# A recurrent attention and two mixing layers on one core: the opening loads, its first and last update of T and K, and its state products rewritten

## The reference

```python
for t in range(S):
    state = alpha[t][:, None] * state + outer(k[t], v[t])   # 48 x 48 per head
    y[t] = q[t] @ state
```

```python
xk = mu_k * x + (1 - mu_k) * x_prev;  xr = mu_r * x + (1 - mu_r) * x_prev
x = sigmoid(xr @ w_r) * (relu(xk @ w_k) ** 2 @ w_v)         # 384 -> 1024 -> 384
u = x + (x^T @ U @ V)^T                                     # over tokens, rank 32
out = u + relu(u @ w_ch1) @ w_ch2                           # 384 -> 1536 -> 384
```

## Time and profile before

| | |
|---|---|
| median of 3 runs | 734.57 us |
| lowest and highest run | 734.43, 735.68 us |
| the profiled execution: its time, its span | 734.48 us, 732.7 us |
| TensorE matmul, share of the span | 96% |
| VectorE, ScalarE, GpSimd | 57%, 35%, 8% |
| DMA, mean over the span | 55 GB/s |

### The profile page before, as it was taken

One profiled execution on the slowest core, in us unless ns is written; L12 is line 12 of the kernel. 1 busy time (PEld: TensorE's weight loads), 2 busy tenths in 40 slices (PEclk: granted clock), 3 DMA queues, 4 the chain that ended last, 5 costly groups with the idle time before them and its releaser, 6 DMA issues.

```text
span 732.7 us, 21764 instructions
## 1 busy us (share of the span) xinstructions
PE 700.2 (96%) x9800; PEld 671.6 (92%) x9800; DVE 416.3 (57%) x731; ACT 259.4 (35%) x516; POOL 62.4 (9%) x123
## 2 busy tenths in 40 slices
PE   4769979999999999999999999999999999999998
PEld 4668968999999999999999999999999998989998
DVE  4788788763874268661885339652685515331312
ACT  1445655324423243243424144243334235321211
POOL 3401101001010011000110010100111000000000
PEclk9969999999999999999999999999999999999999
DMA  8655320023001221024000231023000001000000
GB/s 233 210 196 174 97 86 3 2 90 86 34 4 46 71 59 41 2 58 117 33 4 1 70 105 39 2 59 106 15 32 3 1 10 38 1 1 1 32 1 33
DMA packets 17565, 40.23 MB, mean 55 GB/s; under 512 B 2336, under 2 KB 8480, under 8 KB 17472
## 3 DMA queue, kind: packets, MB, share of 16 engines
q1 hardware_dynamic: 17408, 38.77, 17.5%
q10 hardware_dynamic: 64, 0.07, 0.0%
HBM read 32.93 MB, written 4.72 MB: 51 GB/s over the span
## 4 chain that ended last, share of the span: by engine, by line
PE 90%; DVE 5%; ACT 2%; issue 1%; DMA 1%; SPq 0%; POOL 0%; DVEq 0%; ACTq 0%
PE acc L662 13%; PE hps L662 13%; PE acc L663 13%; PE acc L664 13%; PE hps L664 11%; PE hps L663 11%; PE aps L473 4%; PE aps L636 2%; PE aps L617 2%; PE aps L594 1%; PE aps L484 1%; PE aps L572 1%; DMA QK<-in_q 1%; PE aps L491 1%; DVE QK L1143 1%
## 5 line engine op out<-in xcount | busy, mean ns | idle before, releaser
L1368 DVE SCALAR_TENSOR_TENSOR hid_l<-hps,hid_h 128x384 fp32r<-128x384 f32 x96 | 53.4, 556 | 189.1 <-ACT hid_h L1029 188.6
L1029 ACT ACTIVATE hid_h<-hps 128x384 fp32r<-128x384 f32 x96 | 47.2, 491 | 208.9 <-PE hps L664 208.7
L662 PE MATMUL hps<-in_h,w_h 128*128 128x384 f32 x288 | 98.8, 343 | 0.8 <-DVE in_l L1350 0.8
L664 PE MATMUL hps<-in_h,w_l 128*128 128x384 f32 x288 | 96.9, 336 | 0.0
L663 PE MATMUL hps<-in_l,w_h 128*128 128x384 f32 x288 | 96.8, 336 | 0.0
L663 PE MATMUL acc<-w_l,hid_h 128*128 128x384 f32 x288 | 96.8, 336 | 0.0
L662 PE MATMUL acc<-w_h,hid_h 128*128 128x384 f32 x288 | 96.6, 335 | 0.0
L664 PE MATMUL acc<-w_h,hid_l 128*128 128x384 f32 x288 | 96.4, 335 | 0.0
L1143 DVE TENSOR_TENSOR QK<-QK,T 112x768 f32<-112x768 f32 x80 | 77.0, 971 | 12.4 <-PE aps L473 10.1
L1496 POOL TENSOR_TENSOR T<-T 112x384 f32<-112x384 f32 (+4 forms) x80 | 43.9, 551 | 457.0 <-DVE QK L1143 231.3
L991 ACT ACTIVATE tmp<-hps 128x384 f32<-128x384 f32 x64 | 31.5, 492 | 134.7 <-PE hps L664 134.5
(11 more groups left out here) (134 smaller groups left out, 1228.5 us busy)
## 6 DMA issues: line engine op xcount, KB each, us to landing
QK<-in_k SPq DMA_DIRECT2D x16, 336.0 KB, 4.2
QK<-in_q SPq DMA_DIRECT2D x16, 336.0 KB, 5.2
T<-in_alpha SPq DMA_DIRECT2D x16, 336.0 KB, 4.3
vt<-in_v SPq DMA_DIRECT2D x16, 288.0 KB, 3.2
raw<-in_w_ch SPq DMA_DIRECT2D x6, 768.0 KB, 6.7
out<-x SPq DMA_DIRECT2D x24, 192.0 KB, 1.9
QK<-in_q_odd SPq DMA_DIRECT2D x16, 168.0 KB, 4.1
raw_k<-in_w_k SPq DMA_DIRECT2D x3, 512.0 KB, 4.6
```

The costliest lines, as they stand in the source:

```text
L662: pe.matmul(o, a[0], b[0], start=first, stop=False)
L664: return pe.matmul(o, a[1], b[0], start=False, stop=last)
L1029: nc.scalar.activation(hid[0][:, f % 2, :], hps[f % 2][:, 0:HT], ACT.Relu).then_inc(s_rel2, 1)
L1368: nc.vector.scalar_tensor_tensor(out=hid[1][:, f % 2, :], in0=hps[f % 2][:, 0:HT], scalar=0.0, in1=hid[0][:, f % 2, :].bitcast(F32), op0=A ...
```

## The change

Only the opening (unit 0) is changed, apart from where the low part of V is made.

- The loads of K, Q and T for both g no longer bring the 16 rows between the heads: each of the six is now two of 48 rows, the second head's issued by SyncE and the first head's by ScalarE. VectorE first zeroes rows 32 to 63 of the six tiles, and each of ScalarE's DMAs waits for one of these. The two loads of odd queries become four of 48 rows.
- Level 0 of T is multiplied by VectorE instead of GpSimd.
- The last doubling is four instructions of half the size, K for both g and then Q for both g; `turn_k` waits for K alone, `T_end` for both.
- `end_chunks(0)` goes by the order of the three copies and waits for one at a time; it writes to four banks, one of them of another group, and needs no bank a second time.
- `from_states(0)` waits for 9 of the 11 instructions of `end_states`, that is not for `carry`; the first level of unit 1 waits for all 11.
- One of three copies of the result on VectorE is made by ScalarE, as the last of its own; VectorE's second low part of w_k moves behind its two remaining copies.
- V lands in another place, and its low part is made by VectorE beside the first layer's last step.

```diff
+def first_loads(g):
+    u = units[0]
+    return ((part(u.K(), g), k[0, 0, g], s_ldk[g]), (part(u.Q(), g), q[0, 0, g], s_ldq[g]),
+            (part(u.T[0:HR], g), alpha[0, 0, g], s_lda[g]))
 # SyncE
-            for g in range(2):
-                sp.dma_start(part(K, g), k[0, 0, g]).then_inc(s_ldk[g], 16)
-                sp.dma_start(part(Q, g), q[0, 0, g]).then_inc(s_ldq[g], 16)
-                sp.dma_start(part(T[0:HR], g), alpha[0, 0, g]).then_inc(s_lda[g], 16)
+            for g in range(2):
+                for to, src, done in first_loads(g):
+                    sp.dma_start(to[HS:HR, :], src[HS:HR, :]).then_inc(done, 16)
...
+            sp.wait_ge(s_vst, 3)
             load_part(w2w, w_ch2, 0, F2 // 3, s_w2[2])
 # ScalarE, at its very start
+            for g in range(2):
+                for i, (to, src, done) in enumerate(first_loads(g)):
+                    act.wait_ge(s_zero, 3 * g + i + 1)
+                    act.dma_start(to[0:D, :], src[0:D, :]).then_inc(done, 16)
 # VectorE, at its very start
+            for g in range(2):
+                for to, _, _ in first_loads(g):
+                    nc.vector.memset(to[W2:HS, :], 0.0).then_inc(s_zero, 1)
 # TensorE
             def end_chunks(n):
+                if opens(n):
+                    kept(pe, n, ML, 1)
+                    kept(pe, n, LV, 1)
+                    for j in range(2 * NC):
+                        m, c = j // HC, j % HC
+                        if j % NP == 0:
+                            pe.wait_ge(s_kt, j // NP + 1)
...
             def from_states(n):
-                pe.wait_ge(s_st, st_count(n + 1))
+                pe.wait_ge(s_st, 2 * NT - 3 if opens(n) else st_count(n + 1))
 # VectorE
+            def last_doubles(n):
+                u, l = unit(n), LV - 1
+                for side, of, done in ((left, u.K, s_qk), (right, u.Q, (s_last, s_last))):
+                    for g in range(2):
+                        dve.wait_ge(s_lv[g], (LV - 1) * n + l)
+                        dve.wait_ge(s_T[g], LV * n + l)
...
+                        nc.vector.tensor_tensor(x, x, by, ALU.mult).then_inc(done[g], 1)
...
                         if opens(n):
+                            t_odd, t_even = (x(part(unit(n).T[0:HR], g), 0) for x in (right, left))
+                            dve.wait_ge(s_Ke[g], 1)
+                            nc.vector.tensor_tensor(t_odd, t_odd, t_even, ALU.mult).then_inc(s_T[g], 1)
                             double(n, 0, g)
...
-                nc.vector.tensor_copy(
-                    xT[0:D, 1:KT, 1:1 + HT],
-                    y_all[rows, 2 * HT:].rearrange("p (i t) -> p i t", t=HT)).then_inc(s_xe, 1)
...
                 low(NR)
+                keep_odd(0)
                 low(NR + 1)
-                keep_odd(0)
```

More of the change, by code:

```diff
@@ L197, in ds_block @@
         def ds_block(n, c, z):
+            if opens(n):
+                i, at = (((0, 0), (0, NP * D), (1, 0)), ((2, 0), (2, NP * D), (4, 0)))[z][c]
+                return opening[i][:, at:at + NP * D]
             i, at = (((0, 0), (0, NP * D), (1, 0)), ((1, NP * D), (2, 0), (2, NP * D)))[z][c]
[L199 removed]
+            return aps[i][:, at:at + NP * D]
         def place(y):
@@ L515, in levels @@
                         loaded(pe, n, s_ldk, g)
+                        if g == 0 and n == 1:
+                            pe.wait_ge(s_st, st_count(1))
                         if g == 0 and n == 2:
@@ L606, in own_chunks @@
                 pe.wait_ge(s_kt, kx_count(n + 1))
-                if n > 0:
+                if not opens(n):
                     pe.wait_ge(s_st, st_count(n + 1))
@@ L1143, in double @@
                 nc.vector.tensor_tensor(qk, qk, t, ALU.mult).then_inc(s_qk[g], 1)
+            def last_doubles(n):
[4 more added lines that the diff above has]
+                        dve.wait_ge(s_T[g], LV * n + l)
+                        B, x = 1 << l, side(part(of(), g), l)
+                        t_end = u.T[0:HR, g * S:(g + 1) * S]
+                        at = B - 1 if side is right else 2 * B - 1
+                        by = t_end[:, at:S:2 * B].unsqueeze(2).to_broadcast([HR, S // (2 * B), B])
+                        nc.vector.tensor_tensor(x, x, by, ALU.mult).then_inc(done[g], 1)
             def update_k(n, g):
@@ L1202, in levels @@
                 for l in range(2, LV):
+                    if opens(n) and l == LV - 1:
+                        last_doubles(n)
+                        yield
+                        return
                     for g in range(2):
@@ L1420, in finish_first @@
                 mix(0, 1, 0, lambda: next(first_gate))
-            channel_mix(0, 0, step, FIRST_DVE, finish_first)
+            channel_mix(0, 0, step, FIRST_DVE, finish_first, v_low)
             run(steps)
@@ L1482, in attention @@
                 t = unit(n).T[0:HR]
-                for l in range(LV):
+                for l in range(1 if opens(n) else 0, LV):
                     B = 1 << l
```

57 lines of the change are left out of this document (32 added, 25 removed).

## The result

| | before | after |
|---|---|---|
| median of 9 runs each, same chip | 735.52 us | 737.60 us |
| least, most | 734.43, 737.03 | 735.72, 738.55 |
| profiled execution | 734.48 us (span 732.7) | 735.72 us (span 734.0) |

The ratio is 1.0026, 95% interval 1.0014 to 1.0037: the changed kernel is slower by 0.26%, and the interval lies clear of 1. Forecast were 732.3 us and a range of 730.5 to 733.9.

A forecast was written before the change was run, and what follows sets the result against it. The opening's dependency chain up to the mix was taken as the bound, TensorE being busy and unchanged from 100 us. Terms -0.2 - 0.3 - 0.93 - 0.75 = -2.2 took 734.5 to 732.3 us, range 730.5 to 733.9.

The forecast's parts named there:

- Loads: Opening loads of 96 rows for 112: second Q lands earlier, less zeroing delay; -0.2 us, bounds -1.05 and +0.6.
- rival of slow loads: Opening: twelve 48-row transfers at half rate, second Q landing at 16.9, total 739.6 us; chance 0.05.
- T on VectorE: Opening, level 0: product of T takes 0.57 on VectorE, right behind its update of K; -0.3 us.
- K first and state matmuls by copies: Last doubling to state matmuls: K ready earlier, matmuls no longer wait for third copy; -0.93 us, bounds -0.6 and -1.2.
- Nine instead of eleven: State chain: from_states waits for nine end_states instructions, own_chunks ending at the same moment, 37.5; another -0.75 us.
- third rival: Pause in own_chunks stays at 37.35, ended by something outside the chain; only -0.7, or 733.8 us; chance 0.10.
- Moved copies: Result copies and low parts moved between engines hide in idle time, ScalarE's extra copy under a DMA wait; 0 us.
- The clock: TensorE's granted clock, falling at 38.9 and back at 52.5 in the opening, could change the forecast time.
- first rival: Clock stays at 2.4 GHz through from_states, which saves 1.1; total 731.0 us; chance 0.22.
- second rival: Clock still rises at 52.5, so 2.2 us more of the gate run at half speed; 733.4 us; chance 0.17.
- The test given in the prediction: Mix on VectorE should start at 43.9 instead of 46.06; forecast wrong if it moved by less than 1.5 us.

The follow-up runs named there:

- 48 rows on one queue: Changed kernel with all twelve loads of 48 rows on SyncE, each first head's load behind its zeroing; 735.15 us.
- old loads: Changed kernel with its opening loads as in the kernel before: full 112 rows, all on SyncE, no zeroing; 735.05 us.
- Q before alpha: Changed kernel with old loads, K and Q of both groups issued ahead of both alpha loads; 735.25 us.
- w_v held: Changed kernel with old loads, SyncE's first load of w_v held until own_chunks finished its first group; 734.68 us.
- `end_chunks` as before: Changed kernel with old loads, end_chunks(0) again behind all three copies, in the old order and banks; 735.79 us.
- odd rows behind Q: Changed kernel, SyncE issuing the four odd-query loads only once both halves of the second Q have landed; 737.77 us.
- 32 in front: 32 small matmuls on constants at TensorE's start, spread over four array corners: changed kernel with old loads 733.72 us, kernel before 735.28 us.
- 32 in front, Q first: Changed kernel with old loads and 32 small matmuls at TensorE's start, K and Q of both groups issued ahead of alpha; 733.81 us.

## Why the prediction was wrong

The forecast was 2.2 us faster, and measured were 2.1 us slower. The failed steps are the first, the loads, which alone account for 2.6 of these 4.3 us (-0.2 forecast, +2.4 measured), and the handling of the pause. The other 1.7 are gain that did not come: by the prediction's own sum (Q 2.5 later, less 2.0 of the other steps) 735.0 us was left.

- **Loads, -0.2 (bounds -1.05 and +0.6): wrong.** The second Q came 2.5 later, outside the bounds, and the loads cost 2.4 us alone. The working took the rate of the full rows for the 48 rows and so turned fewer bytes into less time; measured were 205 to 215 GB/s against 260 to 289, so that 48 rows on one queue landed Q at 10.26, full rows at 10.23, and the saving of 1.05 was nothing. It also had SyncE's lead only cancel the saving. With the halves on two queues Q lands 2.1 later than with the same pieces on one, although ScalarE's half was issued 0.4 sooner; 0.6 of that are the odd rows in SyncE's list, and the rest was not separated. The rival of slow loads named this at 0.05; its landing at 16.9 was far off, its sign was right.
- **T on VectorE, -0.3:** as forecast in the rows (0.6 in place of 0.91); too small to be seen in the time.
- **K first and state matmuls by copies, -0.93:** right in the rows. With the pause out of the way, 5.54 became 4.74 (-0.8); with the pause in place it was 4.20 in the changed kernel and 4.58 with old loads.
- **Nine instead of eleven, -0.75:** right where it can act (4.32 became 3.53, -0.79), and void in the changed kernel. The step let the end of `own_chunks` move by 0.93 with its pause of 1.52 unchanged. But the pause ends when a packet of instructions comes, and it was 3.04 long: `own_chunks` resumed 8.0 us behind the transposes before and 7.9 after, as if nothing between them had been shortened. That was the third rival's mechanism (something outside the chain ends the pause), held at 0.10, except that its end did not stay at 37.35. It has no fixed distance to the transposes either: 8.3 with old loads, 6.9 with Q before alpha, 6.1 with w_v held, 10.2 with `end_chunks` as before. The held load shows that the transfers under way set part of it; the rest is open.
- **Moved copies, 0:** nothing in the traces speaks against it. ScalarE's two copies (43.30, 1.60 us) end at 44.9, and its product follows at 44.96, as before (44.87). It follows with no wait, where before it waited 1.62 for the DMA: the cover that the step counted on is used up.
- **The clock:** in the profiled execution it fell later (44.7) and `from_states` took 1.32 as in the first rival, without the gain, since the fetch filled the time; and it came back 4.7 us behind the continuous gate, not 2.9. That part of the second rival (clock returns no earlier) was real: 0.9 us in the profiled execution. In the run nearest to the median, odd rows behind Q, the clock fell at 39.3 and none of the first rival was there.
- **The test given in the prediction**, a mix moved by less than 1.5 us, came out against it: +0.3.

The sum of the old-loads steps was -2.0. By the medians 1.6 of it was there once the pause was moved away (733.72 against 735.28), and 1.2 and 0.7 in the two samples with it in place; the traces don't show it: the earliest gate in any of them is at 49.30 with the steps of before (32 in front), at 49.36 with the changed ones (32 in front, Q first), and at 49.64 before.

## What to carry to other kernels

Before small matmuls in a dense chain are made earlier, count the records from TensorE's start in steps of 128 and see whether a pause with no releaser lies on such a step: what comes earlier may only wait there, and moving the step by a few matmuls of no use can weigh more than the edit, either way (here 32 of them: 2.0 us faster than before, 16: 3.8 slower, none: 1.2 or 0.7 faster). Don't take the time of a transfer of fewer rows from its bytes; time one such transfer first, and look at what each queue sends ahead of the piece that is waited for. And with effects of 0.2% one trace is one execution: look at where it lies among the times of its kernel, and how often each kernel meets which granted clock, before a difference is put down to its code.

## What the runs showed of the hardware

- TensorE's instructions come, by the count and the times of the packets, over the same DMA engines, 16 KB for 128 matmul records, here 3.75 us apart and 2.2 to 3.1 us ahead of the moment at which a pausing TensorE went on; with dense matmuls of 64 columns and a load of 768 KB under way TensorE waited up to 3.2 us (`end_chunks` as before).
- Transfers of 48 rows ran at 205 to 215 GB/s on one queue or two, those of 112 rows at 260 to 289, with the engines counted as busy in both. In the opening the fewer bytes brought no time.
- 128 records of small matmuls (64 rows) in one corner of the array took 0.107 us each, 64 (48 rows) spread over four corners 0.030 (1.94 us in all).
- A memset of 768 columns by 32 rows on VectorE took 0.70 us, as estimated from the 0.11 of 64 columns.
